# Seven block products for x·w_in in the dense steps of an attention + two-layer MLP kernel

## What is computed

```python
scores = scale * q @ k.T;  keep = scores >= max(scores) - tau
x  = softmax(where(keep, scores, -1e9)) @ v          # -> [2304, 512]
h  = x @ w1_in;   x = (h * clip(h + 3, 0, 6) / 6) @ w1_out   # 512 -> 2048 -> 512
h  = x @ w2_in;   y = (h * sigmoid(1.702 * h)) @ w2_out      # 512 -> 2048 -> 512
```

## Time and profile before

| | |
|---|---|
| median of 3 runs | 1128.55 us (1128.35 to 1129.04) |
| profiled execution, own time | 1127.87 us |
| its span in the profile | 1126.0 us |
| TensorE matmuls busy | 1084.6 us, 96% of the span, 6720 matmuls |
| VectorE, ScalarE, GpSimd busy | 559.6, 549.4, 487.7 us |
| DMA moved | 112.37 MB, 100 GB/s on average |

### The profile page before, as it was taken

One profiled execution on the slowest core, in us unless ns is written; L12 is line 12 of the kernel. 1 busy time (PEld: TensorE's weight loads), 2 busy tenths in 40 slices (PEclk: granted clock), 3 DMA queues, 4 the chain that ended last, 5 costly groups with the idle time before them and its releaser, 6 DMA issues.

```text
span 1126.0 us, 17711 instructions
## 1 busy us (share of the span) xinstructions
PE 1084.6 (96%) x6720; PEld 1021.7 (91%) x6720; DVE 559.6 (50%) x1040; ACT 549.4 (49%) x1036; POOL 487.7 (43%) x582
## 2 busy tenths in 40 slices
PE   4888899999999999999999999999999999999998
PEld 3676799999999999999999999989999889999987
DVE  5989878887878887433233222223322222332221
ACT  4888876868686866344334322333322223332221
POOL 3566755545545553384544332144333122222222
PEclk9999999999999999999999999999999999999999
DMA  4447453445343622463233322112221101222210
GB/s 123 118 138 187 118 135 109 122 120 140 111 121 87 169 85 78 115 182 127 89 106 122 122 84 84 41 54 94 94 94 57 56 28 57 85 85 84 84 57 28
DMA packets 91044, 112.37 MB, mean 100 GB/s; under 512 B 25536, under 2 KB 69712, under 8 KB 90960
## 3 DMA queue, kind: packets, MB, share of 16 engines
q1 hardware_dynamic: 90656, 110.96, 33.8%
q10 hardware_dynamic: 304, 0.30, 0.1%
HBM read 78.12 MB, written 33.10 MB: 99 GB/s over the span
## 4 chain that ended last, share of the span: by engine, by line
PE 90%; DVE 4%; issue 3%; ACT 2%; DMA 0%; POOL 0%; SPq 0%; ACTq 0%; POOLq 0%
PE mm L526 20%; PE score L537 17%; PE tr L526 14%; PE score L535 12%; PE score L488 7%; PE tr L503 6%; PE mm L535 6%; PE mm L517 6%; DVE prob L648 2%; DVE neg_max L640 1%; DVE pt_lo L666 1%; ACT pt_hi L775 1%; ACT gate L800 0%; DMA q_raw<-in_qT 0%; ACT prob L770 0%
## 5 line engine op out<-in xcount | busy, mean ns | idle before, releaser
L963 POOL TENSOR_TENSOR g_lo<-act_f,g_hi 128x384 fp32r<-128x384 f32 (+1 forms) x208 | 196.5, 950 | 405.2 <-ACT g_hi L808 405.2
L526 PE MATMUL mm<-x_hi,w_hi 128*128 128x384 f32 (+1 forms) x512 | 162.9, 318 | 0.6 <-DVE x_lo L672 0.5
L526 PE MATMUL mm<-x_hi,w_lo 128*128 128x384 f32 (+1 forms) x512 | 162.2, 317 | 0.0
L526 PE MATMUL mm<-x_lo,w_hi 128*128 128x384 f32 (+1 forms) x512 | 162.1, 317 | 0.0
L775 ACT ACTIVATE pt_hi<-tr 128x640 fp32r<-128x640 f32 x144 | 101.7, 706 | 98.3 <-PE tr L503 97.8
L803 ACT ACTIVATE gate<-mm 128x384 f32<-128x384 f32 x48 | 23.7, 494 | 220.6 <-PE mm L526 220.6
L488 PE MATMUL score<-k_hi,q_sp 128*128 128x288 f32 x320 | 97.7, 322 | 29.3 <-DVE prob L648 20.6
L666 DVE TENSOR_TENSOR pt_lo<-tr,pt_hi 128x640 fp32r<-128x640 f32 x144 | 118.1, 820 | 9.8 <-ACT pt_hi L775 8.8
L640 DVE TENSOR_REDUCE neg_max<-score 128x1 f32<-128x576 f32 x144 | 108.2, 752 | 27.4 <-PE score L488 24.3
L933 POOL TENSOR_SCALAR thresh<-neg_max,tau_abs 128x1 f32<-128x1 f32 x144 | 41.6, 289 | 178.6 <-DVE neg_max L640 178.0
L648 DVE SCALAR_TENSOR_TENSOR prob<-score,thresh,prob 128x576 f32<-128x576 f32 x144 | 116.2, 807 | 0.0
(11 more groups left out here) (82 smaller groups left out, 2463.6 us busy)
## 6 DMA issues: line engine op xcount, KB each, us to landing
x_raw<-x_t_scratch SPq DMA_DIRECT2D x18, 768.0 KB, 6.3
q_raw<-in_qT SPq DMA_DIRECT2D x64, 144.0 KB, 2.8
k_raw<-in_kT SPq DMA_DIRECT2D x62, 144.0 KB, 2.9
stage<-in_w_in SPq DMA_DIRECT2D x16, 512.0 KB, 7.0
stage<-in_w_out SPq DMA_DIRECT2D x16, 512.0 KB, 5.5
o_parts_scratch<-o_t SPq DMA_DIRECT2D x32, 160.0 KB, 1.8
x_t_scratch<-x_raw SPq DMA_DIRECT2D x8, 576.0 KB, 3.4
part_t_scratch<-y_out SPq DMA_DIRECT2D x8, 576.0 KB, 3.5
```

The lines of the kernel that those rows point to most:

```text
L526: m = pe.matmul(bank[:, 0:width], w[:, col:col + P], x[:, k, 0:width], start=(k == 0 and e == 0), stop=(k == KC - 1 and e == 2))
L963: pool.tensor_tensor(g_lo[:, c, 0:width], act_f[:, c % 2, 0:width], g_hi[:, c, 0:width], ALU.subtract).then_inc(g_lo_done, 1)
```

## The change

In steps 1 to 3 the tokens are taken in pairs of 384-token tiles (three pairs a step, nine pairs d = 0 to 8). x of a pair is a 2 x 2 block matrix (halves of the tokens, halves of the 512 features), w_in of the step another (halves of the 512 rows, halves of the 1024 columns). The four blocks of h are made of seven block products, by sums and differences of blocks (Winograd's form), in place of eight. A pair has four groups n of 128 columns of each half of h; a group is seven products of 2 (j) x 3 matmuls of 384 columns, into six PSUM banks in turn. The blocks of h are put together behind the PE:

- ACT copies P1 from PSUM to SBUF (`copy_p1`). DVE adds the other six products with seven additions, each of an SBUF sum and a PSUM bank (`add_c11` to `add_c21`). ACT makes the gates from the sums in SBUF (`gate_of`), DVE multiplies gate and sum, both now in SBUF (`gate_item`), ACT rounds (`high_item`), POOL makes the low part (`low_item`): four blocks C11, C22, C12, C21 of 384 columns per group, through a ring of three.
- For each pair, seven combinations of x blocks are needed in hi and lo. x comes in four pieces of 4 blocks x 192 tokens: `high_pair` (ACT), `low_pair`, `pair_sums` (four additions), `low_pair_sums` (DVE) and `high_pair_sums` (ACT).
- For each step, seven combinations of w_in blocks: eight units of 4 blocks x 128 columns with `high_late_unit` and `high_unit_sums` on ACT, `low_late_unit` on POOL, `unit_sums` on DVE, and the low part of the sums on POOL for even units, on DVE for odd ones. w_out comes in eight more units of 512 columns.
- There is one buffer of weights: combinations of w_in of the next step are made between the last product of a step and the first of the next, beside the last y phase. w_out of a step is brought during the groups of its first pair. The order is in `coming(d)`; DVE empties y blocks in between as `emptied_behind(d)` says.
- The y phase does the same matmuls, as 8 (step 1) or 6 blocks per pair. Output and partial sums go through a ring of three blocks with a DMA for each block, not each tile.
- SBUF is laid out by fixed offsets. `unit_raw` 2 and 3 lie on `act_ring`, 4 to 6 on the sums `sum11`, `sum22`, `sum12`, and so their loads for the next step wait for the step's last item.
- The attention and the tiles of step 0 keep their instructions. In the last two tiles of step 0 the work on the first pair's x and on step 1's units takes the place of the old split of x and units. The unit work now has a DVE part.

Cut to its core:

```diff
+    HIGH_A = ("A11", "A22", "A12", "S3", "S2", "S1", "S4")
+    HIGH_B = ("B11", "B22", "B21", "T3", "T1", "T2", "T4")
+    PRODUCT = {1: ("A11", "B11"), 2: ("A12", "B21"), 3: ("S4", "B22"), 4: ("A22", "T4"), 5: ("S1", "T1"),
+               6: ("S2", "T2"), 7: ("S3", "T3")}
+    PRODUCT_ORDER = (1, 2, 6, 7, 5, 3, 4)
+    GROUPS = FC // 2
+    PRODUCTS = GROUPS * len(PRODUCT_ORDER)
+    BANKS = 6
...
+    ITEMS = [(0, "C11")]
+    for n in range(1, GROUPS):
+        ITEMS += [(n - 1, "C22"), (n - 1, "C12"), (n - 1, "C21"), (n, "C11")]
+    ITEMS += [(GROUPS - 1, "C22"), (GROUPS - 1, "C12"), (GROUPS - 1, "C21")]
...
+        unit_raw = [put(f"unit_raw{i}", at, [P, 4, P]) for i, at in enumerate(
+            (base + 64, base + 2112, base + 4160, base + 6208, at_x + 21504, at_x + 23552, at_x + 25600))]
+        act_ring = put("act_ring", base + 4160, [P, 3, TT])
+        wo_hi = put("wo_hi", at_w, [P, FC, DM], F32R)
+        wo_lo = put("wo_lo", at_w + 16384, [P, FC, DM], F32R)
+        gd_hi = put("gd_hi", at_w + 32768, [P, 2, FC, TT], F32R)
+        y_ring = put("y_ring", at_w + 57344, [P, 3, DM])
...
+        p_bank = h_bank[0:3] + y_bank[0:3]
+        block_bank = {8: [h_bank[3], y_bank[3], p_bank[4], p_bank[5], p_bank[0], p_bank[1], h_bank[3], y_bank[3]],
+                      6: [h_bank[3], y_bank[3], p_bank[4], p_bank[5], h_bank[3], y_bank[3]]}
...
+        def coming(d):
+            if d + 1 == DENSE:
+                return []
+            x = [("x", 4 * max(d + 1, 0) + i) for i in range(4)]
+            units = unit_of(1, 0, 0) if d < 0 else next_units(d)
+            if units is None:
+                return [x[0:2], x[2:4]]
+            w = [("w", units + i) for i in range(2 * GROUPS)]
+            if d < 0:
+                return [x[2:4], w[4:6], w[6:8]] if d == -1 else [w[2:4]]
+            return [x[0:2], w[0:2], x[2:4], w[2:4], w[4:6], w[6:8]]
+        def emptied_behind(d):
+            if d < 0:
+                return [1, 2, 3]
+            if next_units(d) is None:
+                return [3, 5] if blocks_y(d) == 8 else [2, 4]
+            return [0, 2, 4, 5, 6, 7] if blocks_y(d) == 8 else [0, 1, 3, 4, 5, 5]
...
+            def load_late_unit(unit):
+                step, i = 1 + unit // STEP_UNITS, unit % STEP_UNITS
+                _, w_in, w_out, half, _, _, _ = PLAN[step]
+                place = unit_place(unit)
+                raw, loaded = unit_raw[place], unit_loaded[place]
+                if step == 1 and i < 4:
+                    sp.wait_ge(w_lo_done, 4 * UNITS)
+                    sp.wait_ge(inv_turned, PAIRS)
+                    sp.wait_ge(turned, G)
+                elif step > 1 and i < 2 * GROUPS and place in (2, 3):
+                    sp.wait_ge(g_lo_done, STEP0_ITEMS + len(ITEMS) * PAIR_TILES * (step - 1))
+                elif place > 3:
+                    sp.wait_ge(gated_done, len(ITEMS) * PAIR_TILES * (step - 1))
...
+            for d in range(DENSE):
+                units = next_units(d)
+                for b in range(3):
+                    load_part(d, b)
+                if d % PAIR_TILES == 0:
+                    for i in range(2, FC):
+                        load_late_unit(unit_of(dense_step(d), 1, i))
+                if d + 1 < DENSE:
+                    load_pair(4 * d + 4)
+                    load_pair(4 * d + 5)
+                if units is not None:
+                    for i in range(7):
+                        load_late_unit(units + i)
+                if d + 1 < DENSE:
+                    load_pair(4 * d + 6)
+                    load_pair(4 * d + 7)
+                for b in range(blocks_y(d)):
+                    store_block(d, b)
+                    if b > 0:
+                        load_part(d, b + 2)
+                    if b == 2 and units is not None:
+                        load_late_unit(units + 7)
+                if units is not None:
+                    load_late_unit(units + 8)
+                    load_late_unit(units + 9)
+            last = first_block(DENSE) - 1
+            for b in range(last - 2, last + 1):
+                sp.wait_ge(block_stored[b % 3], 16 * on_ring(b))
...
+            def product(d, n, k):
+                p = PRODUCT_ORDER[k]
+                a, b = HIGH_A.index(PRODUCT[p][0]), HIGH_B.index(PRODUCT[p][1])
+                bank = p_bank[(len(PRODUCT_ORDER) * n + k) % BANKS][:, 0:TT]
+                for j in range(2):
+                    for e, (w, x) in enumerate(((ws_hi, xs_hi), (ws_hi, xs_lo), (ws_lo, xs_hi))):
+                        m = pe.matmul(bank, w[:, n, j, b, :], x[j][:, a, :], start=j == 0 and e == 0, stop=j == 1 and e == 2)
+                m.then_inc(made, 1)
+            def bank_free(d, n, k):
+                at = len(PRODUCT_ORDER) * n + k
+                if at >= BANKS:
+                    m, i = divmod(at - BANKS, len(PRODUCT_ORDER))
+                    if i == 0:
+                        pe.wait_ge(p1_copied, GROUPS * d + m + 1)
+                    else:
+                        pe.wait_ge(evicted, 6 * (GROUPS * d + m) + i)
+                elif d > 0 and at < 2:
+                    pe.wait_ge(y_drained, first_block(d - 1) + (5 + at if blocks_y(d - 1) == 8 else 4))
+                elif d == 0 and at > 2:
+                    pe.wait_ge(mm_drained, first_item(TILES) - KC + at - 2)
...
+            for d in range(DENSE):
+                for n in range(GROUPS):
+                    units_split(pe, dense_step(d), 0, n)
+                    if n == 0:
+                        pe.wait_ge(pair_split, 4 * (d + 1))
+                    for k in range(len(PRODUCT_ORDER)):
+                        bank_free(d, n, k)
+                        product(d, n, k)
+                for b in range(3):
+                    dense_block(d, b, 0, GROUPS - 1)
+                for b in range(3):
+                    dense_block(d, b, GROUPS - 1, GROUPS)
+                for b in range(3, blocks_y(d)):
+                    dense_block(d, b, 0, GROUPS)
         @block.vector
...
+            def low_pair(q):
+                _, j, cols = pair_piece(q)
+                dve.wait_ge(pair_hi_done, q + 1)
+                dve.tensor_tensor(xs_lo[j][:, 0:3, cols], pair_raw[:, q % 2, 1:4, :], xs_hi[j][:, 0:3, cols], ALU.subtract
+                                  ).then_inc(pair_lo_done, 1)
+            def pair_sums(q):
+                a21, a11, a22, a12 = (pair_raw[:, q % 2, i, :] for i in range(4))
+                dve.wait_ge(pair_lo_done, q + 1)
+                dve.tensor_tensor(a22, a21, a22, ALU.add).then_inc(pair_s1_done, 1)
+                dve.tensor_tensor(a21, a11, a21, ALU.subtract).then_inc(pair_s1_done, 1)
+                dve.wait_ge(pair_s1_done, 3 * q + 2)
+                dve.tensor_tensor(a11, a22, a11, ALU.subtract).then_inc(pair_s1_done, 1)
+                dve.wait_ge(pair_s1_done, 3 * q + 3)
+                dve.tensor_tensor(a12, a12, a11, ALU.subtract).then_inc(pair_sums_done, 1)
+            def low_pair_sums(q):
+                _, j, cols = pair_piece(q)
+                dve.wait_ge(pair_sums_hi_done, q + 1)
+                dve.tensor_tensor(xs_lo[j][:, 3:7, cols], pair_raw[:, q % 2, :, :], xs_hi[j][:, 3:7, cols], ALU.subtract
+                                  ).then_inc(pair_split, 1)
+            def unit_sums(unit):
+                w = 2 * GROUPS * (unit // STEP_UNITS) + unit % STEP_UNITS
+                b12, b11, b22, b21 = (unit_raw[unit_place(unit)][:, i, :] for i in range(4))
+                dve.wait_ge(unit_lo_done, w + 1)
+                dve.tensor_tensor(b11, b12, b11, ALU.subtract).then_inc(unit_t_done, 1)
+                dve.tensor_tensor(b12, b22, b12, ALU.subtract).then_inc(unit_t_done, 1)
+                dve.wait_ge(unit_t_done, 3 * w + 2)
+                dve.tensor_tensor(b22, b22, b11, ALU.subtract).then_inc(unit_t_done, 1)
+                dve.wait_ge(unit_t_done, 3 * w + 3)
+                dve.tensor_tensor(b21, b21, b22, ALU.subtract).then_inc(unit_sums_done, 1)
+            def low_unit_sums(unit):
+                n, j = divmod(unit % STEP_UNITS, 2)
+                dve.wait_ge(unit_sums_hi_done, 2 * GROUPS * (unit // STEP_UNITS) + unit % STEP_UNITS + 1)
+                dve.tensor_tensor(ws_lo[:, n, j, 3:7, :], unit_raw[unit_place(unit)][:, :, :], ws_hi[:, n, j, 3:7, :], ALU.subtract
+                                  ).then_inc(unit_split[unit_place(unit)], 1)
+            def bring(two):
+                for what, i in two:
+                    if what == "x":
+                        low_pair(i)
+                for what, i in two:
+                    if what == "x":
+                        pair_sums(i)
+                    else:
+                        unit_sums(i)
...
+            def gate_item(d, n, which, bank):
+                k = item(d, n, which)
+                place = act_ring[:, k % 3, :]
+                dve.wait_ge(gate_done, k + 1)
+                if dense_step(d) == 1:
```

(81 more changed lines are left out.)

700 lines of the change are left out of this document (471 added, 229 removed).

## The result

The changed kernel takes 1122.35 us (median of 5 runs, 1120.75 to 1123.72), beside 1128.35 for the kernel before in the same job: ratio 0.9949 [0.9935, 0.9964]. It is faster, by 6.0 us where 19 to 20 were forecast, and lies 2.35 us above the range. The profiled execution took 1121.46 us, its span 1119.7.

What follows compares the result with a forecast made beforehand. The prediction took TensorE, 96% busy, as the bound: 1127.87 - 37.4 (fewer matmuls) + 6.5 (seam) + 2 (pair 0) + 9 (two boundaries) = 1108.0 us, forecast 1108 to 1109, range 1094 to 1120.

Steps and rivals of the forecast that it cites:

- The saving: Products of steps 1 to 3: 24 fewer matmuls a pair, 4.16 us each over nine pairs, 37.4 us.
- the pace of the seven products: Steps 1 to 3: a product lasts 1.04 us, a group 7.28, a pair's products 29.1 us.
- the boundary model: Boundaries before steps 2 and 3: next w_in and x work outlasts the y phase, PE loses 4.5 us each, 9 for two.
- ACT's copy of P1 the releaser: Start of step 2 and 3 products: PE gaps of 3 to 6 us, this copy and DVE's first addition last.
- The step that failed: First pair of a step: banks and y work of three groups hide w_out's lag if DVE starts on time; nothing charged.
- POOL's 1.2 us a group: First pair of a step: w_out's low parts put POOL and DVE behind by this, 4 to 5 us in the pair.
- Rival 2: Boundaries heavier, 9 to 12 us each, first pair's lag adding 2 to 4: 1119, 1115 to 1125 us; chance 0.18.
- Rival 1: Steps 1 to 3: all added work is hidden, 1090.5 to 1097 us; chance 0.17.
- Rival 3: DVE becomes the bound, each gate multiplication waiting for a whole POOL operation: 1158 us; chance 0.07.
- Pair 0's start: Step 1's first products: DVE ready 2 us late for the reuse of P2's bank, 2 us (0 to 4).
- The seam: Last two tiles of step 0: x and unit work delays gate multiplications and low parts, 6.5 us (0 to 10).
- The lower bound of 5.0 us for a pair of units: Step boundaries: at 5.0 us per two w_in units, not 6.2, the PE loses 0.

Runs made afterwards that it cites:

- the best version: Changed kernel with w_out's units half a place earlier, w_in's and w_out's low parts on DVE, w_out's first two units loaded earlier: 1096.32 us, again 1096.96 us.
- the first run: w_out's units brought half a place earlier in a step's first pair, against the changed kernel: 1119.85 us, 0.9919.
- the earlier loads alone: Only w_out's first two units of a step loaded ahead of the last y block's store, against the changed kernel: 1118.86 us, 0.9924.

## Why the prediction missed

**What held.** The saving, 37.4 us, and the pace of the seven products. Pairs 1, 2, 4, 5, 7 and 8 without a gap. Much of the boundary model: DVE ready 42.7 us after the y phase began, for 43.4 forecast; a pair of units in 6.42 us, for 6.2; ACT's copy of P1 the releaser.

That the products of pairs 3 and 6 lost 5.0 and 4.5 us, for 4.5 each, is partly luck. In pair 3 the stop at the banks cost 2.9 us: the eighth product began 10.1 us in, where 11.6 was forecast. The other 2.0 us are later waits for additions, forecast as absorbed. In pair 6 the stop cost 2.9 us too, and the lower clock behind it, which the forecast had not, 1.6.

**The step that failed** is the one that charged nothing for w_out: "The banks and the 9.4 (step 1) or 12.3 us of y work of the first three groups take that up if DVE starts on time." It is wrong in two ways. First, the y work of three groups is not the slack of the unit that binds. `dense_block` takes a block's columns group by group, so the third group's, with units 4 and 5 of w_out, are wanted after 12 matmuls: 2.1 us (step 1) or 2.7 us into the y phase. In POOL's order unit 5 stands behind the last group's C11. The run with w_out's units earlier moved it in front and had whole y phases, with DVE as late as before.

Second, its condition was false by the prediction's own sum, which had DVE 10.1 us late at each boundary, and late at pair 0. The slack of the banks was spent twice, on DVE's late start and on POOL's 1.2 us a group. The groups of pair 3 took 8.0 to 8.6 us for the 7.28 of their products, as these first additions show (the first group's is at 740.96):

```profile
749.00 0.54 DVE L1051 TENSOR_TENSOR sum<-sum,tr 128x384 f32<-128x384 f32 x1
757.64 0.54 DVE L1051 TENSOR_TENSOR sum<-sum,score 128x384 f32<-128x384 f32 x1
765.69 0.54 DVE L1051 TENSOR_TENSOR sum<-sum,score 128x384 f32<-128x384 f32 x1
```

The low part came too late for y: 4.2, 2.2 and 1.9 us, 8.3 in all for 0 charged, and the 2.0 us of additions in pair 3 come on top. The run without w_in shows that nothing is lost in steps 2 and 3 when DVE is on time. Rival 2 had 2 to 4 us for this lag, and the time fell within its 1115 to 1125, but not by its mechanism: it had 9 to 12 us at a boundary, and the products lost 5.0 and 4.5. Rival 1, all hidden, did not come for this kernel; the best version above, at 1096.3 to 1097.0, reaches its range.

The row behind it, from the timeline of after: three gate multiplications with POOL idle, then three while it is busy.

```profile
698.94 1.49 DVE L1038 SCALAR_TENSOR_TENSOR act_ring<-act_ring,sum 128x384 f32<-128x384 f32 x3
```

```profile
753.15 2.86 POOL L1525 TENSOR_TENSOR wo_lo<-unit_raw,wo_hi 128x512 fp32r<-128x512 f32 x2
753.97 3.75 DVE L1040 TENSOR_TENSOR act_ring<-act_ring,sum 128x384 f32<-128x384 f32 x3
755.98 2.59 POOL L1533 TENSOR_TENSOR gd_lo<-act_ring,gd_hi 128x384 fp32r<-128x384 f32 x2
```

1.49 us against 3.75: they alternate with POOL's operations, one for one. The Trainium skill (SBUF — State Buffer, Who interferes with whom) states such an exclusive hold, and the trace agrees. The prediction summed it properly, as a sum of both engines' times, and then left that sum out of the total. Rival 3, the rule applied to every gate, did not come: the mean gate multiplication of steps 2 and 3 is 737 ns in after, 0.15 us over the 587 ns with a lighter POOL, and pairs 1, 2, 4 and 5 have no gap. But in a step's first pair it came in part: 3.75 us for three is 1.25 each, near its 1.46.

**Mis-sized terms.** Pair 0's start: 4.9 us for 2 (0 to 4), of which 2.77 is one wait and about 1.6 the clock, below. The seam: 8.3 us for 6.5, within its bounds of 0 to 10; 2.3 of them fall in tile 6, which had 1 in the forecast. With w_in's low parts on DVE alone the seam is 1.9 us shorter and pair 0's products lose nothing. The lower bound of 5.0 us for a pair of units was no bound for that version, which takes 4.72: it took POOL's part as given and asked only how badly it collides.

## What to carry to other kernels

When slack hides two things, charge it once: a term set at nothing "if the engine is on time" has to be looked up again after the sum has said when that engine is on time. Take slack from the first instruction that needs the late piece, not from the length of the phase: here 2.1 or 2.7 us, not 9.4 or 12.3. Where two engines exclude each other, their times add, so splitting a chain of dependent SBUF operations between them bought nothing here: it went faster whole on the engine that does it faster, although that one was the busier. And before a small gain is read from the whole time, compare the stage that was changed: the first run's 6.5 us showed as 2.5.

## What the runs showed of the hardware

The granted clock fell to its lower level, 1.2 GHz, behind three of after's waits. The window over such a stretch:

```profile
545.00:548.00 3.00, 2.97 (x10) 2.97 (x11) 2.60 (x6) 1.14 (x2) 0.00 (x0) 0.56 0.80 251
```

Matmuls of 384 columns start 0.32 us apart there (575.09 and 575.41 above) instead of 0.173, some ten each time, about 1.6 us. So such a wait cost over half as much again. In after it came behind PE waits of 2.77, 2.43 and 2.72 us, and not behind those of 2.08, 2.03 and 1.49. But the length of the wait does not decide it. At the same place in pair 3's y phase the clock fell behind a wait of 1.96 us in the kernel with the earlier loads alone, and of 1.84 us in the one with w_in's low parts on DVE, where after's 2.03 left it. And the best version's two profiles have the same four waits in the last y phase of step 0 (0.80, 0.41, 0.18 or 0.19, 0.40 or 0.41 us), and the clock fell in one of them only, which made that phase 1.5 us longer. The first, then the second:

```profile
523.00:526.00 3.00, 3.00 (x25) 3.00 (x24) 2.51 (x8) 0.85 (x2) 0.00 (x0) 1.00 0.71 213
523.00:526.00 3.00, 3.00 (x15) 3.00 (x14) 2.64 (x9) 0.85 (x2) 0.00 (x0) 0.51 0.76 223
```

No run here isolates what decides it.

DVE's fp32 subtraction with all operands in SBUF takes 0.69 us for 512 columns with no collision. POOL's takes 1.3 us (at 746.43 us in after), and 1.45 on average in the same place, collisions included. The run that moved w_out's low parts went the way of that ratio and not of the engines' busy shares.
